# A chunked linear recurrence: outputs and state increments on column quarters of the TensorE array instead of halves

## The reference

```python
f = 1.0 / (1.0 + np.exp(-f_logit))             # batch 4, heads 8, seq 768, head_dim 48
state = np.zeros((B, H, D, D))
for t in range(S):
    state = f[:, :, t, :, None] * state + np.einsum('bhd,bhe->bhde', k[:, :, t], v[:, :, t])
    y[:, :, t] = np.einsum('bhd,bhde->bhe', q[:, :, t], state)
```

## Time and profile before

| | |
|---|---|
| median of 3 runs | 587.57 us (587.3 to 587.59) |
| the profiled execution | 587.03 us, its span 585.3 us |
| instructions | 13946 |
| TensorE matmul, weight load | 546.2 us busy (93%), 511.0 us busy (87%), 5916 records each |
| VectorE, ScalarE, GpSimd | 371.7, 298.9 and 131.6 us busy |
| TensorE's granted clock | full in each of the 40 slices |

### The profile page before, as it was taken

One profiled execution on the slowest core, in us unless ns is written; L12 is line 12 of the kernel. 1 busy time (PEld: TensorE's weight loads), 2 busy tenths in 40 slices (PEclk: granted clock), 3 DMA queues, 4 the chain that ended last, 5 costly groups with the idle time before them and its releaser, 6 DMA issues.

```text
span 585.3 us, 13946 instructions
## 1 busy us (share of the span) xinstructions
PE 546.2 (93%) x5916; PEld 511.0 (87%) x5916; DVE 371.7 (63%) x672; ACT 298.9 (51%) x599; POOL 131.6 (22%) x88
## 2 busy tenths in 40 slices
PE   0999988999889998899999899999999999999997
PEld 0789777998778897789987799999999999999997
DVE  3978888678778687755767667554345634354324
ACT  5768687665857548732568565223332424133311
POOL 2012044045500014300033138212210222013110
PEclk9999999999999999999999999999999999999999
DMA  8938012062210340000800000011000100010002
GB/s 290 337 116 295 2 37 75 3 226 84 72 29 3 115 185 1 2 2 8 319 2 2 1 1 1 1 41 41 2 0 28 55 0 1 9 63 12 2 0 82
DMA packets 17969, 37.24 MB, mean 64 GB/s; under 512 B 2160, under 2 KB 10608, under 8 KB 17392
## 3 DMA queue, kind: packets, MB, share of 16 engines
q1 hardware_dynamic: 17904, 36.32, 17.8%
HBM read 31.46 MB, written 4.72 MB: 62 GB/s over the span
## 4 chain that ended last, share of the span: by engine, by line
PE 80%; DVE 9%; ACT 6%; issue 2%; DMA 1%; SPq 1%; DVEq 0%; ACTq 0%
PE bank L1188 18%; PE bank L1189 18%; PE bank L1190 17%; ACT prob L699 4%; PE bank L1325 4%; PE bank L1392 4%; PE bank L1286 3%; PE bank L1351 3%; PE bank L1206 3%; PE bank L1282 2%; DVE probT L1094 2%; PE bank L1267 2%; PE bank L1253 2%; DMA OT<-w_theta 1%; PE bank L1483 1%
## 5 line engine op out<-in xcount | busy, mean ns | idle before, releaser
L1188 PE MATMUL bank<-z_h,wt_h 128*128 128x384 f32 x288 | 97.8, 339 | 0.0
L1189 PE MATMUL bank<-z_l,wt_h 128*128 128x384 f32 x288 | 97.4, 338 | 0.0
L1190 PE MATMUL bank<-z_h,wt_l 128*128 128x384 f32 x288 | 96.5, 335 | 0.0
L699 ACT ACTIVATE prob<-bank,nmax 128x384 f32<-128x384 f32 (+5 forms) x96 | 60.0, 634 | 22.1 <-DVE nmax L1074 22.1
L505 POOL TENSOR_TENSOR trig<-trig,x 128x768 f32<-128x768 f32 x18 | 33.5, 1863 | 152.0 <-ACT trig L615 92.6
L1074 DVE TENSOR_REDUCE nmax<-bank 128x1 f32<-128x384 f32 (+5 forms) x96 | 54.9, 616 | 9.6 <-ACT prob L699 6.1
L927 DVE TENSOR_SCALAR turns<-bank 128x384 int32<-128x384 f32 x22 | 12.2, 556 | 72.9 <-PE bank L1190 72.9
L1188 PEld LDWEIGHTS bank<-z_h,wt_h 128*128 128x128 f32 x288 | 54.0, 188 | 0.6 <-issue 0.2
L1189 PEld LDWEIGHTS bank<-z_l,wt_h 128*128 128x128 f32 x288 | 54.1, 188 | 0.0
L1190 PEld LDWEIGHTS bank<-z_h,wt_l 128*128 128x128 f32 x288 | 54.0, 188 | 0.0
L803 ACT CAST uT_h<-bank 128x384 fp32r<-128x384 f32 x24 | 11.5, 478 | 81.0 <-PE bank L1483 81.0
(11 more groups left out here) (177 smaller groups left out, 1411.6 us busy)
## 6 DMA issues: line engine op xcount, KB each, us to landing
V<-v SPq DMA_DIRECT2D x4, 1152.0 KB, 11.4
gate<-fT SPq DMA_DIRECT2D x12, 384.0 KB, 3.2
q<-qT SPq DMA_DIRECT2D x12, 384.0 KB, 6.6
k<-kT SPq DMA_DIRECT2D x12, 384.0 KB, 7.4
wt_raw<-w_tok SPq DMA_DIRECT2D x6, 768.0 KB, 9.6
out<-x SPq DMA_DIRECT2D x24, 192.0 KB, 1.9
gate<-fT SPq DMA_DIRECT2D x3, 512.0 KB, 5.1
q<-qT SPq DMA_DIRECT2D x3, 512.0 KB, 9.4
```

Source lines behind the costliest of these rows:

```text
L699: nc.scalar.activation(prob[:, m % 2, r, at], bank[r][:, at], ACT.Exp, bias=nmax[:, m, k:k + 1], accum_out=den[:, m // 2, which, e:e + 1]) ...
L1188: nc.tensor.matmul(o, a_h, b_h, start=start, stop=False)
L1189: nc.tensor.matmul(o, a_h, b_l, start=False, stop=False)
L1190: return nc.tensor.matmul(o, a_l, b_h, start=False, stop=stop)
```

## The change

Both functions address the array's columns in four quarters of 32. In `outputs` each product is issued four times with a quarter of the weights each. In `increments` each head has two matmuls of 32 weight columns, the even head on quarters 0 and 1, the odd head on 2 and 3. The streamed operand, the columns streamed per matmul, the order of the groups, the waits and the semaphores stay as they are.

```diff
                     for p in range(PAIRS):
-                        for h in range(2):
-                            at = slice((2 * p + h) * HD, (2 * p + h + 1) * HD)
-                            mm = nc.tensor.matmul(ps(6)[64 * h:64 * h + 64, at],
-                                                  kTs[:, c % 2, p * P + 64 * h:p * P + 64 * h + 64],
+                        for n in range(4):
+                            at = slice((2 * p + n // 2) * HD, (2 * p + n // 2 + 1) * HD)
+                            mm = nc.tensor.matmul(ps(6)[32 * n:32 * n + 32, at],
+                                                  kTs[:, c % 2, p * P + 32 * n:p * P + 32 * n + 32],
                                                   V[:, c, at], start=True, stop=True)
                     mm.then_inc(inc_done, 1)
...
-                    halves_of = [slice(0, 64), slice(64, P)]
+                    quarters = [slice(32 * n, 32 * n + 32) for n in range(4)]
                     for h in range(H):
                         if c >= 1 and h % 2 == 0:
-                            for own in halves_of:
+                            for own in quarters:
                                 nc.tensor.matmul(ps(4 + c % 2)[own, h * HD:(h + 2) * HD],
                                                  q[:, h // 2, c * P + own.start:c * P + own.stop],
                                                  S[:, c % 2, h // 2, :], start=True, stop=False)
-                        for own in halves_of:
+                        for own in quarters:
                             mm = nc.tensor.matmul(ps(4 + c % 2)[own, h * HD:(h + 1) * HD],
                                                   Am[:, c % 2, slot(h) // P, own], V[:, c, h * HD:(h + 1) * HD],
                                                   start=(c == 0), stop=(c == 0 or h % 2 == 1))
```

## The result

The changed kernel takes **598.5 us** (median of 4 runs, 596.66 to 603.03), the kernel before beside it 587.58 (4 runs, 587.3 to 588.9): ratio 1.0188, 95% interval 1.0155 to 1.0222. That is 10.9 us slower, where 4.9 faster was forecast. The profiled execution took 598.99 us with a span of 597.3, so it lies 11.96 above the profiled one of before (587.03). The remaining 1.0 us is how far those two executions lie from their medians, 0.5 us each.

A forecast was written before the change was run, and what follows sets the result against it. The prediction took TensorE, busy 93% of the span, as the bound where stages wait for it. Batches save 0 + 1.6 + 1.6 + 1.8 = 5.0 us, less 0.1: 587.57 - 4.9 = 582.7 us, range 581.0 to 588.0.

The forecast's parts named there:

- Items 1 and 2: Touched matmuls: 1,408 more records, same number of rounds; a 48-column round takes 0.042 us instead of 0.058, 8.8 us of TensorE time.
- rule of 60 cycles: Skill's rule against splitting: overhead of 25 ns per record would make an outputs with state 2.4 us against 1.6.
- rival A: Four quarters do not run at once, two wait for the other two: slower, 612 us; chance 19%.
- C: Rival: 18 ns of a round are a fixed cost of each pass, so no effect, 587.5 us; chance 7%.
- Item 3: Savings on the path over the four batches: 5.0 us, less 0.1 for staggered starts, gain 4.9 us.
- Batch 0, gain 0: In batch 0 the chain runs over VectorE and ScalarE, not TensorE, so nothing is saved there: 0 us.
- chunk 0 and the last outputs: Savings per batch: chunk 0 gives 0.2 us in batches 1 and 2, 0.39 in batch 3; last outputs 0.26 each.
- The wait before the last outputs: Sign: TensorE's idle time there grows from 0.24 to about 0.6 us in batches 1 to 3.
- Item 4: TensorE's queue must hand out a load with its matmul every 11 to 14 ns; taken to cost nothing.
- Item 5: Instruction fetch for 2,816 more loads and matmuls, 0.18 MB more: costed at nothing, hidden by nearly idle DMA engines.
- rival B: Queue hands out a load with its matmul every 15 ns: only 2.1 us gained, 585.5 us; chance 10%.
- The clock: TensorE's granted clock is 1.0 in these stretches and was to stay at 2.4 GHz.

The follow-up runs named there:

- e13: Changed kernel, quarters only in batches 1 to 3, for the first outputs with first increments and the last outputs; median 1.4 us below the kernel before, gain 0.17%.
- e1: Changed kernel with only increments on quarters, outputs on halves as before; its time is not in the text, only that it was above the expected 586.3 us.
- e6: Changed kernel, quarters only in batches 1 to 3 and not in step 4, rest on halves; time not in the text, it missed the expected 583.5 to 586.
- e10: Changed kernel, quarters only in batches 1 to 3, for increments and two of four pairs of heads; not faster than the kernel before, time not in the text.
- e7: Changed kernel, all quarters, with two of batch 1's four gate loads issued after batch 0's recurrence; total did not move from the changed kernel's, time not in the text.
- e4: Changed kernel with increments and two of four pairs of heads on quarters in all batches; time not in the text, above the expected 584.5 to 587 us.

## Why the prediction was wrong, point by point

*Items 1 and 2, counts and rounds: right.* 7,324 records, 1,536 and 640 and 640; loads of 112 ns (113 forecast); a pair of heads 0.34 (0.335), increments 0.36 (0.37), first outputs 0.70 (0.70), a step 3.50 (3.48). The estimate of a 32-column load, below the stream's 40 ns, held. So did the reading of two L1286 starts within 0.02 us against the rule of 60 cycles for each matmul ("TensorEngine Tiling (Array Packing)" of the Trainium skill, Performance Considerations). 24 records in 0.34 us are 14 ns each, for four tiles; by that rule it would have been 25. Rivals A and C fall with it.

*Item 3, what lies on the path: right where it could be seen.* With the fetch kept out of the way, e13's three batches gave 0.42, 0.41, 0.61. By the prediction's terms chunk 0 and the last outputs are worth 0.46, 0.46, 0.65. "Batch 0, gain 0" was not put to a test of its own, and batch 0 was not thereby safe: it is where most of the loss is, since VectorE's cover hides a faster TensorE, not one that stops for 3.5 us. It was to end its recurrence when it does now and ends it 3.9 us later (46.51 for 42.65). The wait before the last outputs, which was to grow from 0.24 to 0.6, is gone: behind the stalls TensorE is the late one.

*Item 4, handing out: right as far as it went.* At most 8.4 ns for each instruction within a piece that is there. The two starts of rows 4 measured the sequencer with its instructions at hand.

*Item 5, code: the step that failed.* It read "Costed at nothing; the nearly idle DMA engines hide it." I took the share of 0.5% for the price. That is a figure of bandwidth, and the fetch is bound by its turn: 3.3 to 3.9 us for each 16 KB, one piece at a time. Half of what shows this was in the profile of before: 0.77 MB in 47 packets are 16 KB each, 256 instructions, and the step of 3.48 us that I had worked out would hold 296. I never set 256 instructions against the length of a packet's turn. That length was not to be had from rows 1: 0.5% of 16 engines over the span is 1.0 us for a packet, and the rest of the turn shows only where TensorE stalls. And "it would act as in 4" would have priced it wrongly too: 14 ns for an instruction are 28 ns for a load with its matmul, and at 25 ns rival B already has rival A's time, 612 us. In truth what is inside a piece runs at full speed, lighter groups (scores, turns) make up for dense ones within a piece, and only the deficit of a whole piece comes, as one stop. The right question was how long the queue takes for each run of 256 instructions: 1.7 to 2.2 us where increments and outputs fill it, against 3.3 to 3.9.

*The clock: wrong for three of the four executions.* In the profiled one 1.2 GHz followed the stall in batch 0 for 3.4 us, and the wait behind it for another 3.4; one execution kept 2.4 GHz throughout.

*Range and chances.* 598.5 lies outside 581.0 to 588.0; slower had 0.19, all of it on rival A, four quarters taking turns, which did not happen. A rival on the side of slower was there, but not its mechanism.

**Open.** Why TensorE waits 1.8 us instead of 0.4 at L1420 at the end of batch 0 when that batch is late (VectorE's and ScalarE's part of the tail is later too) was not taken apart; ScalarE's last copy of xn (L685) starts at 48.02 there, behind two gate activations (L514) of which the second waited 0.64 us for VectorE. Nor was the half clock near 79 us in e1, e6 and e10 (82 in e7), 3.4 us long and some 1.4 us of time, which the profiles of before and after do not have. It need not come from quarters: of the 87 executions of the kernel before beside the experiments 18 were granted 0.997 or less, and they took 588.1 to 592.7. How the stalls differ from run to run is not known, only the one profiled execution of each.

## What to carry to other kernels

Splitting these fp32 matmuls over four column tiles cost the array nothing, and each split doubles the instructions: before doing it, count the instructions of an engine and ask of every run of 256 how long it lasts. Where that was under the fetch's turn of here 3.3 to 3.9 us, this engine stopped at the 256th instruction, wherever in the code that was; spend the split where it gives most for each instruction, and keep it out of stretches already dense. An idle wait called "issue" in the middle of a group that has no wait there is the sign, and large loads beside such a stretch lengthened it (3.20 us idle, 1.28 with half of the loads later).

## What the runs showed of the hardware that was not expected

- TensorE's instructions come 256 at a time, 16 KB, in 3.3 to 3.9 us when little else moves, in about 5.7 behind 1.1 MB of loads (35.40 to 41.14).
- The piece ahead is the only reserve: the lighter step before the last outputs did not keep them from stalling (e6, 0.49 us idle at 123.28).
- Changing the tile width from 32 to 64 columns in a stream costs some 0.11 us (e1, e4), which can be all that the narrower tiles gained.
- A stop of TensorE of 3.2 us was paid twice in the profiled execution: the clock granted afterwards was 0.50 for 3.4 us.
